# End of batch 0's body: maxima, residual sums, k's load and kmax's trip in another order

## The reference

```python
q_s = softmax(q, over the 64 columns of a head)      # q - max, exp, / sum
k_s = softmax(k, over the 576 tokens)                # k - max over tokens, exp, / sum
x   = q_s @ (k_s^T @ v)                              # attention, per head
h   = gelu(x @ w_in);  u, v = halves(h)
v_n = (v - mean(v)) / sqrt(var(v) + 1e-6) * g_ln
x1  = x + (u * (w_sg @ v_n + b_sg)) @ w_out          # residual
h   = relu(x1 @ w_in2)
out = (h * sigmoid(conv3(h, conv_w))) @ w_out2
```

## Time and profile before

| | |
|---|---|
| median of 3 runs | 946.67 us (946.52 to 947.38) |
| the profiled execution, its own time | 948.56 us |
| its span, first to last instruction | 946.8 us |
| mean granted TensorE clock | 0.991 |
| PE busy | 923.9 us, 98% |
| PE weight load, DVE, ACT, POOL busy | 91%, 64%, 40%, 38% |
| DMA | 77.84 MB, mean 82 GB/s |

### The profile page before, as it was taken

One profiled execution on the slowest core, in us unless ns is written; L12 is line 12 of the kernel. 1 busy time (PEld: TensorE's weight loads), 2 busy tenths in 40 slices (PEclk: granted clock), 3 DMA queues, 4 the chain that ended last, 5 costly groups with the idle time before them and its releaser, 6 DMA issues.

```text
span 946.8 us, 14688 instructions
## 1 busy us (share of the span) xinstructions
PE 923.9 (98%) x5980; PEld 864.1 (91%) x5980; DVE 601.5 (64%) x943; ACT 374.9 (40%) x564; POOL 361.9 (38%) x230
## 2 busy tenths in 40 slices
PE   6899899999999999999999998999999999999998
PEld 5799799899999998999999997999998989999987
DVE  6667666657746666576355797866667666667660
ACT  3561433524524335245234254533434333434331
POOL 4985545446426444464204133322222222232320
PEclk8899999999999999999999999999999999999999
DMA  8815425134061151330412302020202020200001
GB/s 256 251 48 178 134 51 193 37 100 158 12 200 56 45 194 41 99 109 12 134 64 82 111 13 73 12 84 23 73 23 73 23 73 23 84 23 22 25 23 55
DMA packets 50482, 77.84 MB, mean 82 GB/s; under 512 B 4336, under 2 KB 22768, under 8 KB 49520
## 3 DMA queue, kind: packets, MB, share of 16 engines
q1 hardware_dynamic: 45808, 67.48, 22.6%
q10 hardware_dynamic: 4608, 9.44, 2.7%
HBM read 56.97 MB, written 18.89 MB: 80 GB/s over the span
## 4 chain that ended last, share of the span: by engine, by line
PE 89%; DVE 6%; DMA 2%; issue 1%; ACT 1%; POOL 1%; SPq 0%; ACTq 0%; DVEq 0%; POOLq 0%
PE psum L452 51%; PE psum L444 29%; PE psum L510 3%; PE psum L593 2%; PE psum L486 2%; PE psum L545 1%; DMA plain_arena<-in_q 1%; DVE plain_arena L1322 1%; DVE split_arena L1304 1%; DMA x_dram<-plain_arena 1%; DVE plain_arena L1133 0%; DVE plain_arena L1246 0%; DVE split_arena L1462 0%; DVE plain_arena L1320 0%; DVE plain_arena L1215 0%
## 5 line engine op out<-in xcount | busy, mean ns | idle before, releaser
L452 PE MATMUL psum<-split_arena 128*128 128x288 f32 x4032 | 559.0, 297 | 6.0 <-DVE split_arena L1201 2.9
L452 PEld LDWEIGHTS psum<-split_arena 128*128 128x128 f32 x4032 | 545.9, 189 | 12.6 <-DVE split_arena L1201 3.2
L444 PE MATMUL psum<-split_arena 128*128 128x512 f32 x1248 | 298.3, 393 | 2.7 <-DVE split_arena L1462 2.6
L444 PEld LDWEIGHTS psum<-split_arena 128*128 128x128 f32 x1248 | 232.2, 189 | 49.8 <-DVE split_arena L1462 3.5
L1614 POOL TENSOR_TENSOR plain_arena<-plain_arena 128x576 f32<-128x576 f32 x64 | 107.4, 1678 | 281.6 <-ACT plain_arena L915 281.6
L1325 DVE SCALAR_TENSOR_TENSOR plain_arena<-plain_arena 128x576 f32<-128x576 f32 x64 | 96.2, 1503 | 2.2
L1320 DVE TENSOR_SCALAR plain_arena<-plain_arena 128x576 f32<-128x576 f32 x64 | 36.0, 563 | 90.1 <-ACT plain_arena L909 90.1
L1555 POOL TENSOR_TENSOR plain_arena<-plain_arena 128x576 f32<-128x576 f32 x32 | 46.5, 1453 | 110.6 <-DVE plain_arena L1259 110.6
L909 ACT ACTIVATE plain_arena<-psum 128x576 f32<-128x576 f32 x64 | 41.6, 650 | 105.4 <-PE psum L452 74.4
L915 ACT ACTIVATE plain_arena<-plain_arena 128x576 f32<-128x576 f32 x64 | 43.7, 683 | 43.5 <-DVE split_arena L1462 40.4
L1462 DVE TENSOR_TENSOR split_arena<-plain_arena,split_arena 128x576 fp32r<-128x576 f32 x64 | 53.2, 832 | 10.9 <-ACT split_arena L921 10.0
(11 more groups left out here) (80 smaller groups left out, 787.0 us busy)
## 6 DMA issues: line engine op xcount, KB each, us to landing
x_dram<-plain_arena ACTq DMA_DIRECT2D x32, 288.0 KB, 2.1
plain_arena<-x_dram SPq DMA_DIRECT2D x8, 1152.0 KB, 5.7
out_rows<-plain_arena SPq DMA_DIRECT2D x36, 256.0 KB, 2.0
plain_arena<-in_v SPq DMA_DIRECT2D x32, 256.0 KB, 3.3
plain_arena<-in_kT SPq DMA_DIRECT2D x7, 1152.0 KB, 8.0
plain_arena<-in_q SPq DMA_DIRECT2D x7, 1024.0 KB, 5.7
plain_arena<-in_k SPq DMA_DIRECT2D x7, 1024.0 KB, 5.6
plain_arena<-in_w_in SPq DMA_DIRECT2D x8, 512.0 KB, 5.8
```

The lines of the kernel that those rows point to most:

```text
L444: mm = e.matmul(out, stat[s], mov[m], start=first and n == 0, stop=last and n == 2, skip_group_check=True)
L452: mm = e.matmul(out[:, h, 0:NH], stat[s], mov[m][:, h * NH:(h + 1) * NH], start=first and n == 0, stop=last and n == 2, skip_group_check=True)
```

## The change

- POOL: `sub_k(1, 0)` moves from between the first two `inverse_deviation` steps of body 0 to behind the last `lo_vn`; `sub_k(1, 2)` moves behind `gate(0, 0)`. At the end of body 0, `sub_k(2, 0)` moves between `sub_q(2, 0)` and `sub_q(2, 1)`.
- ACT: `exp_k(1, 2)` moves behind `hi_q(1, 0)`.
- DVE: at the end of body 0, `max_q(2, 0)` moves from ahead of the four `add_x` to behind `lo_x(1, 0)`, and `max_q(2, 1)` and `max_q(2, 2)` behind `lo_x(1, 1)`.
- SP: `spread_kmax(2)` goes ahead of `load_k(2)`, and `load_k(2)` waits also until the first x1 store has landed.

```diff
--- before.py
+++ after.py
@@ -385,11 +385,11 @@
                     load_v(n, 1)
                     load_q(n)
                     if isinstance(m, int) and m == 0:
+                        spread_kmax(n)
                         e.wait_ge(q_in, 32 * n)
+                        e.wait_ge(x1_out[0], 16)
                     load_k(n)
                     load_v(n, NJ - 1)
-                    if isinstance(m, int) and m == 0:
-                        spread_kmax(n)
 
             body(0, 2)
             for i in range(1, B - 2):
@@ -1002,14 +1002,15 @@
                 if start:
                     for u in range(NU):
                         exp_q(a, u)
-                    for u in range(NU):
-                        exp_k(a, u)
+                    exp_k(a, 0)
+                    exp_k(a, 1)
                     for w in range(len(W_OUT)):
                         hi_late(W_OUT, w_out_raw, w_out_hi, w)
                 for f in range(FT):
                     if start:
                         if f == 1:
                             tile(0)
+                            exp_k(a, 2)
                             tile(1)
                         elif f == 2:
                             tile(2)
@@ -1427,8 +1428,6 @@
                 if start:
                     max_k(n, 0)
                     max_k(n, 1)
-                    max_q(n, 0)
-                    max_q(n, 1)
                 elif n is not None:
                     max_q(n, 0)
                     max_q(n, 1)
@@ -1441,13 +1440,16 @@
                 if a is not None:
                     lo_x(a, 0)
                 if start:
-                    max_q(n, 2)
+                    max_q(n, 0)
                 if a is None:
                     set_edges()
                     convolve(0, 0)
                 add_x(m, 3)
                 if a is not None:
                     lo_x(a, 1)
+                if start:
+                    max_q(n, 1)
+                    max_q(n, 2)
 
             first_attention()
             body(0, 1, 2)
@@ -1576,28 +1578,29 @@
                     for u in range(NU):
                         scale_q(a, u)
                 inverse_deviation(m, 0)
-                if start:
-                    sub_k(a, 0)
                 inverse_deviation(m, 1)
                 lo_vn(m, 0)
                 inverse_deviation(m, 2)
                 lo_vn(m, 1)
                 lo_vn(m, 2)
                 if start:
+                    sub_k(a, 0)
                     sub_k(a, 1)
-                    sub_k(a, 2)
                     scale_q(a, 0)
                 for f in range(FT):
                     gate(m, f)
                     if start and f == 0:
+                        sub_k(a, 2)
                         scale_q(a, 1)
                         scale_q(a, 2)
                     if start and f < 2:
                         lo_w_out(f)
                 if n is not None:
                     sub_q(n, 0)
+                    if start:
+                        sub_k(n, 0)
                     sub_q(n, 1)
-                    for u in range(NU):
+                    for u in range(1 if start else 0, NU):
                         sub_k(n, u)
                     sub_q(n, 2)
```

## The result

The changed kernel takes 954.26 us (median of 6 runs, 952.04 to 955.65); the kernel before, on the same chips, 947.02 us (6 runs, 945.44 to 948.98). The ratio is 1.0068, with a 95% interval of 1.0054 to 1.0082. By that ratio it is 6.4 us slower (the two medians are 7.2 us apart), where 2.2 us were forecast, and it lies outside the range given. The profiled execution has a span of 953.1 us (before 946.8) and a mean clock of 0.987 (before 0.991).

A forecast was written before the change was run, and what follows sets the result against it. PE, busy 98% of the span, was taken as the bound, so only its stops counted. +1.0 us at `x_piece(1, 3)` plus 1.2 us of slow clock made 946.67 + 2.2 = 948.9 us, range 944.8 to 951.0.

The forecast's parts named there:

- Part 1, the 0.6 us in front: With `sub_k(1, 0)` moved, DVE's normalisation and `lo_vn` come 0.6 us earlier; PE's 0.56 us stop near 64 goes.
- Part 1, POOL's row of work: POOL runs 1.85 us later up to `lo_w_out(1)`; PE stops 1.2 us near 81 and 0.6 near 86, ending 1.7 behind.
- Part 2: End of body 0: residual sums ahead of `max_q`, store landing in 2.5 us; `x_piece(1, 1)` at 98.5, 2.9 us won.
- rival D: The x1 store lands in 4.9 us instead of 2.5, k's load 2.4 us later: 951.3 us, chance 0.11.
- Part 3: `hi_x` waits behind ACT's exponentials: stops of 2.1 and 3.4 us ahead of `x_piece(1, 2)` and `(1, 3)`, the latter at 111.2.
- The clock: The granted clock falls again around the new stops near 110 us, costing 1.2 us, from a span of nothing to 1.6.
- The sum: PE reaches `x_piece(1, 3)` 1.0 us later, plus 1.2 us of slow clock: +2.2 us in all.
- Rival A: The same stops with no slow clock behind them: +1.0 us, 947.7 us, chance 0.20.
- B: `lo_g(0, 1)` slips in between POOL instructions, no 1.2 and 0.6 us stops: 945.9 us without slow clock, chance 0.17.
- C: The gain comes through: stops of 1.59 and 2.92 us and the slow clock go, 6.1 us, to 940.6; chance 0.07.

The follow-up runs named there:

- e7: Kernel before with only the first half, `sub_k(1, 2)` placed behind `scale_q(1, 2)` and `exp_k(1, 2)` one tile later on ACT: 947.99 us against 947.32, ratio 1.0002.
- e1: Kernel before with only the first half (`sub_k(1, 0)`, `sub_k(1, 2)` and `exp_k(1, 2)` moved): 951.22 us against 948.10, ratio 1.0042.
- e2: Kernel before with only the second half, the changes at the end of body 0: 951.61 us against 948.10, ratio 1.0038.
- e3: Changed kernel with `sub_k(1, 2)` and `exp_k(1, 2)` back in their old places: 953.12 us against 948.10, ratio 1.0055.
- e4: e2 with ACT's order changed, `hi_x` of body 1 ahead of the exponentials of batch 2: 946.86 us against 948.10, ratio 0.9990.
- e11: Changed kernel with `sub_k(1, 2)` behind `scale_q(1, 2)` and `exp_k(1, 2)` behind `hi_q(1, 1)`: 952.93 us against 947.66, ratio 1.0056.
- e5: e4 with the read of kmax moved behind the x1 store and k's load: 946.40 us against 947.32, ratio 0.9994.
- e12: Changed kernel with e7's place for `sub_k(1, 2)`, e4's ACT order and e5's late read of kmax: 946.86 us against 947.66, ratio 0.9993.
- e8: Kernel before with only `sub_k(1, 2)` and `exp_k(1, 2)` moved, `sub_k(1, 0)` in its old place: 948.66 us against 947.32, ratio 1.0014.
- e9: e5 without SP's wait for the x1 store ahead of k's load: 950.03 us against 947.69, ratio 1.0023.

## Why the prediction was wrong

The sign was right, and so were the two stops behind the moved `max_q`. The size was not, +2.2 us forecast and +6.4 measured, nor the first place: the stops forecast near 81 and 85.5 did not come, and one of 3.05 us ahead of `turn_q(1, 2)` stood in their stead.

- **Part 1, the 0.6 us in front**: right. DVE's small instruction (L1221, before L1220) takes 0.16 us instead of 0.75, the stop at L593 is gone. The trace agrees here with the Trainium skill, page "SBUF — State Buffer", section "Who interferes with whom": the DVE instruction had been held by POOL's.
- **Part 1, POOL's row of work**: the step that failed. I followed the delay of POOL to `lo_g(0, 1)`, "All behind it keep their lengths", and took `lo_g(0, 0)` to be as long as before. It took 6.28 us instead of 1.65: with `sub_k(1, 2)` ahead of the `scale_q`, DVE missed its turn at three ends of POOL instructions. PE stopped 3.05 us, the slow clock cost 1.7 us more, and `o_part(0, 0)` was 4.3 us late; forecast were 1.7. Where `lo_g(0, 0)` is let in (e7), the two small stops are 0.95 and 0.34 us for my 1.2 and 0.6. e1 prices the half at 0.42%.
- **Part 2**: right in what it removes, both stops went. The 2.5 us for the store came true (2.2) by luck: the delay had put the read of kmax 2.35 us ahead of it. Issued just behind that read it takes 4.5 us and more (e2, e3, e4, e11), near the 4.9 that I had given to rival D and put down to k's load. In those runs k's load is not yet issued, and e5 shows that it was kmax's read. For the 4.9 us of the kernel before, where k's load is issued 4.0 us ahead of the store and kmax's read 3.7 us behind it, no run separates the two.
- **Part 3**: the mechanism was right and e4 shows it by taking it away. The stops were 1.70 and 3.99 us for 2.1 and 3.4. k's load took 7.1 us for my 6.3. With that and the store 2.2 us later than forecast, `x_piece(1, 3)` came at 113.98 for my 111.2.
- **The clock**: the term was mis-sized. I took 1.2 us for one fall; it was 2.6 us behind the last stop, with the clock at 1.2 GHz from 112.6 to 119.4, on top of 1.7 us at 78 that the sum did not have. The length of a stop did not give the size. Behind the last stop it was 1.7 us in e2 (3.01 us of stop) and e11 (3.55), and 2.7 in e3 (3.30). Ahead of `x_piece(1, 1)` a stop of 2.18 us was followed by 12 matmuls in 4.50 us in e3 and in 2.93 in e4.
- The sum: 3.8 us at `x_piece(1, 3)` and 2.6 us of slow clock behind it are 6.4 us, for my 1.0 and 1.2. The errors do not simply add: with `lo_g(0, 0)` let in (e11) the store takes 4.5 us in place of 2.2, the stop ahead of `x_piece(1, 1)` is there, and 5.3 us of loss are left. So the store and the clock were wrong terms too, the store's hidden behind the first error.
- Rival A (no slow clock) is out; so is B (the backlog hidden), as `lo_g(0, 1)` took 2.18 us again; C needed ACT's order changed, and even with it (e4, e12) no more than 1 us came of the 6, as the store, kmax's read and gelu stepped in.
- The range was too narrow on the slow side: its ends took one late step at a time, but there were three new stops, and the two longest each brought a spell of slow clock.

## What to carry to other kernels

When work is moved on POOL, go through every VectorE instruction with two SBUF inputs in the stretch that it moves into, not only the one that was held before, and look for gaps in POOL's row where it can get in. Small ones count too: `sum_q` on 64 x 8 elements was held to 2.24 us in e8. When a step is taken off one engine's path, check first what the in-order engine behind it (here ACT, with `hi_x` behind `exp_q`) will then have to wait for: repairing that order was worth 4.75 us (e4 against e2). A store on which a wait hangs should have no larger read issued just ahead of it from another queue.

## What the runs showed of the hardware

- A VectorE subtraction that waited from 70.15 us was passed over at three successive ends of POOL instructions and took 6.28 us (6.27 in e1); in another order it was let in at the first end, in an unbroken row, and took 1.73 us (e7, e11). What decides this is open, and it is not tied to the 64-row subtraction: e3, e4, e5 and e12 have such passes behind 128-row instructions. The traces point to how much of the running POOL instruction was left at the issue. Of the `TENSOR_TENSOR` and `TENSOR_SCALAR` instructions of DVE, in all 14 traces, that were held by a POOL instruction with another close behind it, the 125 with 1.0 us or more left were let in at its end (112 of them are one repeated step, `normalise`, with 2.1 us left). Of the 25 with less, 10 were passed over and 15 were not (11 of these had 0.5 us of a `gate` left). Nine of the ten got in only where POOL itself had to wait. No run varied the time left alone.
- The same x1 store landed in 2.1 us with nothing beside it (e5), 2.2 us when the 256 KB read of kmax was 2.35 us ahead, 4.6 us when that read was 0.2 us ahead (e4), and 7.5 us behind that read and k's load (e9).
- The write of kmax, 2 KB, landed in 1.4 us with an idle queue, and in 6.0 us behind k's load in the kernel before.
